# A fused mLSTM and gated feed-forward kernel on Trainium2: gate rows reordered for fewer transfers, and the first units rearranged

## The chip, the cores and the metric

The kernel runs on one core of one Trainium2 chip. The metric is the device time of the program in microseconds (us). Engines are named as in the profile: PE is TensorE (matmuls), DVE is VectorE, ACT is ScalarE, POOL is GpSimd, SP is SyncE, which here only issues DMAs. PE's clock has two levels in the profile: a granted clock of 1.00 is 2.4 GHz, 0.50 is 1.2 GHz.

## The reference

A gated linear attention (mLSTM) over 2 batches, 8 heads, 768 positions, head size 40, followed by two gated feed-forward layers with 320 model columns and 1536 hidden columns:

```
m_new = max(f + m, i);  f_stab = exp(f + m - m_new);  i_stab = exp(i - m_new)
C = f_stab * C + i_stab * v k^T;   n = f_stab * n + i_stab * k
y = sigmoid(o) * (C q) / max(|n.q|, 1)
x = y in token order, 1536 x 320
x = (silu(xn @ w_gate) * (xn @ w_val)) @ w_out      with xn = x / rms(x) * rms_g
x = (sigmoid(x @ w_gate2) * (x @ w_val2)) @ w_out2
```

All of it is in float32.

## The kernel before

**Tiles.** Time is cut into 6 chunks of 128 positions; with 2 batches this makes 12 attention tiles t of 128 tokens x 8 heads. Within a chunk the recurrence is written as matmuls: the exponents of the decay matrix come from one matmul of `lhs` (rows a) and `rhs` (rows log, spread over 4 heads), ACT takes the exponential into `prob`, PE makes the scores q k^T, DVE multiplies (`weigh_scores`), and PE multiplies with v (`outputs`). A state per batch is carried from chunk to chunk. `normalise(t)` divides and applies the output gate, `sum_squares` (ACT), `root` (POOL, a power of -0.5) and `scale_y` or `early_scale` make the normed x, `turn_x` (PE) transposes it, and `round_x` (ACT) and `rest_x` (DVE) split it in a high part `x_hi` and a rest `x_lo`.

**Gate rows.** The gates' prefix sums and maxima run along the free dimension, with one (batch, head) pair a partition: 16 rows, and a second copy of them for chunk 0. Each value goes into the exponent matmul as high part and rest. The gates are handled in three parts (`PARTS`): chunk 0, chunk 1, and chunks 2 to 5, which are copied to other partitions (`m_q`, `fi_q`, "late rows") so that one instruction handles four chunks. Their results come back by DMA: `load_lhs` writes a's rows into `lhs`, `load_rows(j)` the log rows of half tile j into one of four `rhs` buffers.

**Units.** The feed-forward work is cut into 78 units u, each 128 hidden columns by 256 or 512 tokens. In a unit PE runs `gate_products(u)`, `value_products(u)` and `result_products(u - 1)`; ACT applies the activation (`activate`) and rounds the hidden values (`round_hidden`); DVE does `gate_hidden` (units of the first two blocks), `value_hidden`, `rest_hidden`. PE starts gate_products(u + 1) only when `gate_hidden(u)` has read the bank. Units 0 to 11 have 256 tokens. Tiles 0 and 1 are made ahead of unit 0; tiles 2 to 11 are woven into the units: `SCORE_AT` starts tile 2 at unit 0, tile 3 at unit 2, tile 4 at unit 9, tile 5 at 11 and so on; `OUT_AT` is one unit later.

**Order.** No scheduler: each engine's order is that of the code, and semaphores join the engines. Each engine takes its instructions strictly in order, so one that waits holds up all behind it. `G2` is a table of the units at which the five steps for the late rows stand: stabiliser(2) on DVE; late_differences on POOL and the mask rows on ACT; late_sums and round_late; late_exponentials and late_rests; late_decays. SP's loads of them follow a unit later (`G2[0] + 1`, `G2[3] + 1`). `WARM` holds how many matmuls on a constant tile (`keep_clock_up`) stand at ten places ahead of unit 0.

**PE ahead of unit 0**: filling matmuls; scores(0); scores(1); early_exponents(0) to (3); early_outputs(0) to (3); turn_x(0); turn_x(1); turn_gates(0); filling matmuls between them.

Of the kernel before, what the change touches and what calls it, by code (L numbers as in the profile page):

```python
# [12 lines left out]
F32 = mybir.dt.float32  # L13
F32R = mybir.dt.float32r
# [52 lines left out]
LATE = B * H * (CH - C2)  # L67
EARLY = 8
G2 = (2, 4, 5, 5, 6)
WARM = (12, 0, 2, 0, 0, 5, 2, 4, 2, 1)  # L70
# [7 lines left out]
def pattern(j):  # L78

    return HG * (2 * (j // 2 % B) + j % 2)  # L80
# [22 lines left out]
def build(nc, qk1, k1, v1, og, fi_in, fi_late, gains, const, masks, wgv1, wo1, wgv2, wo2, outT):  # L103
    with ExitStack() as ctx:
# [27 lines left out]
        ones = sb("ones", [LATE, ROWS])  # L132
# [3 lines left out]
        is_a, is_log = consts[0:GATES, C_A:C_A + 1], consts[0:GATES, C_LOG:C_LOG + 1]  # L136
# [3 lines left out]
        with rows:  # L140
# [5 lines left out]
            c_gate = sb("c_gate", [B * H, CH], F32, rows)  # L146
            c_diag = sb("c_diag", [B * H, CH, B, H], F32, rows)
            log_early = sb("log_early", [ROWS, L], F32, rows)
            r_row = sb("r_row", [GATES, C2, L], F32, rows)
# [3 lines left out]
            c_q, diag_q = sb("c_q", [LATE, 1], F32, rows), sb("diag_q", [LATE, LATE], F32, rows)  # L153
            a_split = sb("a_split", [2 * LATE, L], F32, rows)
# [5 lines left out]
        with att:  # L160
# [9 lines left out]
            log_rows = sba("log_rows", [ROWS, 1, L])  # L170
            log_split = sba("log_split", [2 * LATE, L])
# [6 lines left out]
            gate = [sba(f"gate{p}", [P, H, D]) for p in range(2)]  # L178
            den, rden = sba("den", [P, H]), sba("rden", [P, H])
            y1 = sba("y1", [P, H, D])  # L180
            ssq, msq, rstd = (sba(n, [P, 2]) for n in ("ssq", "msq", "rstd"))
# [3 lines left out]
            mask_l = y_tail[ROWS:P, 0:2 * L].rearrange("p (m s) -> p m s", m=2)  # L185
# [12 lines left out]
        xt_ps = lambda t: (bank[4], bank[1])[t] if t < B else bank[7]  # L198
        cols_ps = lambda p: bank[7][:, H * DV + (2 * B * H if p == 1 else 0):]
# [5 lines left out]
        fi_late_in, m_late_in, ones_in, lhs_in = (sem(n) for n in ("fi_late_in", "m_late_in", "ones_in", "lhs_in"))  # L205
# [9 lines left out]
        m_done, kl_own, kl_done, log_done, a_own, a_done, log_hi_done, log_lo_done, a_hi_done, a_lo_done, w_done = (  # L215
            sem(n) for n in ("m_done", "kl_own", "kl_done", "log_done", "a_own", "a_done", "log_hi_done",
                             "log_lo_done", "a_hi_done", "a_lo_done", "w_done"))
        lhs_const, rhs_const, sel_const, setup_pool, im_done, exps_done, cols_turned, cols_done, diag_done, rhs_own, act_own = (
            sem(n) for n in ("lhs_const", "rhs_const", "sel_const", "setup_pool", "im_done", "exps_done", "cols_turned",
                             "cols_done", "diag_done", "rhs_own", "act_own"))  # L220
# [6 lines left out]
        gate_done, den_done, rden_done, y1_done, y_done, ssq_done, msq_done, rstd_done, xn_done = (  # L227
            sem(n) for n in ("gate_done", "den_done", "rden_done", "y1_done", "y_done", "ssq_done",
                             "msq_done", "rstd_done", "xn_done"))
# [18 lines left out]
        def _(sp):  # L248
# [7 lines left out]
            def load_rows(j):  # L256
# [7 lines left out]
                for n in range(2):  # L264
                    src = log_rows[GATES * n + at:GATES * n + at + HG, 0]
                    if c >= C2:
                        at_late = LATE * n + B * H * (c - C2) + at
                        src = log_split[at_late:at_late + HG]
                    sp.dma_start(rhs[i][GATES * n + B * H:GATES * n + B * H + 1].bitcast(F32),
                                 src).then_inc(rows_in[i], 16)  # L270

            def load_m_late():

                sp.wait_ge(m_done, 3)
                m = m_row[0:B * H].rearrange("p c s -> p (c s)")
                for c in range(C2, CH):
                    at = B * H * (c - C2)
                    sp.dma_start(m_q[at:at + B * H], m[:, L * c - 1:L * c + L]).then_inc(m_late_in, 16)
# [1175 lines left out]
```

## Time and profile before

| | |
|---|---|
| three timed runs | 494.49, 494.61, 496.36 us; median 494.61 us |
| profiled execution, its own time | 497.38 us |
| its span on the core | 495.6 us |
| mean granted clock | 0.985 |
| busy | PE 478.5 us (97%), DVE 228.3, ACT 185.8, POOL 29.9 |
| DMA | 26.08 MB, mean 53 GB/s |

PE is the engine to look at. Its busy time is modelled from the starts of pipelined matmuls, so its share says little alone; the stretches where it is idle, or where the granted clock is 0.50, are what can be won. A row of a timeline gives start, duration, engine, line, operation, output and inputs, and in square brackets the engine's idle time before it with what ended it.

### The profile page before, as it was taken

To read this page: it belongs to the slowest core of one execution; us is meant where nothing else is said; L and a number is where in the kernel's file an instruction comes from. 1 tells how busy PE (TensorE), PEld (TensorE's weight loads), DVE (VectorE), ACT (ScalarE), POOL (GpSimd) and SP (SyncE) were. 2 spreads that over 40 slices of the span, in tenths; PEclk is the share of its full clock that TensorE was granted. 3 is DMA by queue.
4 is the path that set the end of the run, shared out by engine and by line. 5 is a ranking of instruction groups with operands and counts; after the bars stand their busy time and mean duration, and the time that the engine had idled before them with its cause. 6 is when DMAs were issued, how large, how long until landed. Compare 5 with 4: busy or idle time off the path is not lost.

```text
span 495.6 us, 7191 instructions
## 1 busy us (share of the span) xinstructions
PE 478.5 (97%) x2700; PEld 397.9 (80%) x2702; DVE 228.3 (46%) x452; ACT 185.8 (37%) x386; POOL 29.9 (6%) x69
## 2 busy tenths in 40 slices
PE   8799889999999999999999999999999999999996
PEld 4599879888878877878888888888888888888884
DVE  4768736667555544454555545222232222322222
ACT  6645523554354242334545455122232212222221
POOL 3421101111101000000000000000000000000000
PEclk8979989999999999999999999999999999999999
DMA  6354215542020130000232320000010000100001
GB/s 206 124 154 136 82 22 170 159 128 67 1 69 18 37 118 0 2 1 1 63 117 91 92 76 0 2 0 1 0 54 1 0 1 0 54 1 0 1 1 53
DMA packets 15795, 26.08 MB, mean 53 GB/s; under 512 B 2448, under 2 KB 10736, under 8 KB 15760
## 3 DMA queue, kind: packets, MB, share of 16 engines
q1 hardware_dynamic: 15536, 25.50, 17.0%
q8 instruction: 21, 0.34, 0.3%
q10 hardware_dynamic: 224, 0.12, 0.1%
q14 instruction: 14, 0.11, 0.1%
HBM read 23.40 MB, written 1.97 MB: 51 GB/s over the span
## 4 chain that ended last, share of the span: by engine, by line
PE 57%; issue 34%; POOL 3%; DVE 2%; DMA 1%; ACT 1%; SPq 1%; POOLq 0%; ACTq 0%
PE bank L1257 37%; PE bank L1308 5%; PE bank L1310 5%; PE bank L1309 5%; PE bank L1316 2%; PE bank L1317 2%; POOL vw L438 1%; DMA qk_tile<-qk 1%; POOL msq L452 1%; POOL faded L445 1%; POOL rstd L455 1%; PE bank L1150 0%; PE bank L1191 0%; PE pair L1191 0%; DVE hid_lo L984 0%
## 5 line engine op out<-in xcount | busy, mean ns | idle before, releaser
L1257 PE MATMUL bank<-x_hi,gv_split 128*128 128x512 f32 (+1 forms) x780 | 242.1, 378 | 2.9 <-DVE x_lo L939 1.8
L1257 PE MATMUL bank<-x_lo,gv_split 128*128 128x512 f32 (+1 forms) x468 | 175.1, 377 | 0.0
L1257 PEld LDWEIGHTS bank<-x_hi,gv_split 128*128 128x128 f32 x780 | 145.6, 192 | 30.0 <-issue 3.8
L1257 PEld LDWEIGHTS bank<-x_lo,gv_split 128*128 128x128 f32 x468 | 89.7, 192 | 14.9
L582 ACT ACTIVATE hid_hi<-hid 128x512 fp32r<-128x512 f32 (+1 forms) x78 | 46.7, 599 | 140.4 <-DVE hid L977 90.5
L977 DVE TENSOR_TENSOR hid<-hid,bank 128x512 f32<-128x512 f32 x48 | 33.0, 688 | 132.4 <-PE bank L1257 132.4
L575 ACT ACTIVATE hid<-bank 128x512 f32<-128x512 f32 (+1 forms) x78 | 43.9, 562 | 112.5 <-PE bank L1257 112.4
L984 DVE TENSOR_TENSOR hid_lo<-hid,hid_hi 128x512 fp32r<-128x512 f32 (+1 forms) x78 | 51.3, 658 | 52.1 <-ACT hid_hi L582 52.1
L1308 PE MATMUL bank<-hid_hi,wo_split 128*128 128x512 f32 (+1 forms) x156 | 60.8, 389 | 0.4 <-DVE hid_lo L984 0.4
L1310 PE MATMUL bank<-hid_hi,wo_split 128*128 128x512 f32 (+1 forms) x156 | 58.3, 374 | 0.0
L1309 PE MATMUL bank<-hid_lo,wo_split 128*128 128x512 f32 (+1 forms) x156 | 58.3, 374 | 0.0
L1308 PEld LDWEIGHTS bank<-hid_hi,wo_split 128*128 128x128 f32 x156 | 29.4, 188 | 6.8 <-DVE hid_lo L984 0.8
L964 DVE SCALAR_TENSOR_TENSOR hid<-hid,bank 128x512 f32<-128x512 f32 (+1 forms) x30 | 17.4, 579 | 37.0 <-ACT hid L575 37.0
L1310 PEld LDWEIGHTS bank<-hid_hi,wo_split 128*128 128x128 f32 x156 | 29.4, 188 | 5.3
L1309 PEld LDWEIGHTS bank<-hid_lo,wo_split 128*128 128x128 f32 x156 | 29.4, 188 | 4.6
L1316 PE MATMUL bank<-hid_hi,wo_split 128*128 128x512 f32 (+1 forms) x78 | 29.2, 374 | 0.0
L1317 PE MATMUL bank<-hid_lo,wo_split 128*128 128x512 f32 (+1 forms) x78 | 29.1, 373 | 0.0
L973 DVE SCALAR_TENSOR_TENSOR hid<-hid,bank 128x512 f32<-128x512 f32 (+1 forms) x30 | 17.4, 580 | 22.3 <-PE bank L1257 21.6
L948 DVE TENSOR_TENSOR gv_split<-gv_raw,gv_split 128x768 fp32r<-128x768 f32 x24 | 23.2, 967 | 3.0 <-ACT gv_split L561 3.0
L1201 PEld LDWEIGHTS pair<-v_sb,prob 128*128 128x128 f32 x160 | 18.9, 192 | 0.4
L1201 PE MATMUL pair<-v_sb,prob 128*128 128x42 f32 x160 | 18.9, 279 | 0.0
L532 ACT ACTIVATE hsum<-gate 128x320 f32<-128x320 f32 x12 | 5.7, 474 | 29.8 <-DVE gate L923 29.8
(147 smaller groups left out, 376.3 us busy)
## 6 DMA issues: line engine op xcount, KB each, us to landing
gv_raw<-wgv SPq DMA_DIRECT2D x24, 384.0 KB, 3.1
qk_tile<-qk SPq DMA_DIRECT2D x24, 160.0 KB
wo_raw<-wo SPq DMA_DIRECT2D x24, 160.0 KB, 3.1
v_sb<-v SPq DMA_DIRECT2D x12, 168.0 KB, 4.3
gate<-og SPq DMA_DIRECT2D x12, 160.0 KB, 3.1
k_sb<-k SPq DMA_DIRECT2D x10, 160.0 KB, 4.3
outT<-y_out SPq DMA_DIRECT2D x6, 256.0 KB, 2.0
rhs<-log_split SPq DMA_DIRECT2D x32, 2.0 KB
```

The costliest lines, as they stand in the source:

```text
L575: ins = nc.scalar.activation(hid[j][:, 0:size], g_ps[:, 0:size], func, scale=0.5 if tanh else 1.0)
L582: nc.scalar.activation(hid_hi[j][:, 0:size], hid[j][:, 0:size], ACT.Copy).then_inc(hi_done, 1)
L948: nc.vector.tensor_tensor(wgv[f][:, :, 3:6], raw[:], wgv[f][:, :, 0:3].bitcast(F32), ALU.subtract).then_inc(gv_ready, 1)
L977: ins = nc.vector.tensor_tensor(h, h, v_ps[:, 0:size], ALU.mult)
L984: nc.vector.tensor_tensor(hid_lo[j][:, 0:size], hid[j][:, 0:size], hid_hi[j][:, 0:size].bitcast(F32), ALU.subtract).then_inc(lo_done, 1)
L1201: pe.matmul(pv_ps(2 * t + g)[:, DV * h:DV * h + DV], prob[t % 2][:, g, h], v_sb[t % 3][:, HG * g + h], start=True, stop=True)
L1257: mm = pe.matmul(ps[:, 0:size], lhs, rhs, start=(i == 0), stop=(i == len(passes) - 1))
L1308: pe.matmul(out, w_hi, hi, start=first, stop=False)
L1309: pe.matmul(out, w_hi, lo, start=False, stop=False)
L1310: mm = pe.matmul(out, w_lo, hi, start=False, stop=last)
L1316: pe.matmul(out, w_end, hi, start=first, stop=False)
L1317: mm = pe.matmul(out, w_end, lo, start=False, stop=last)
```

## The change

It reorders the gate rows, moves steps between engines, and moves steps along each engine's order. The arithmetic of the reference stays, with another split of the rounding.

1. **Gate rows.** The rows are now 32 (`GATES`) in four groups of (batch, half of the heads), and each group has its 4 heads twice: once for the a or log row's high part, once for its rest. So the two parts of a half tile stand next to each other, and `load_rows(j)` issues one DMA instead of two, `load_lhs` four instead of eight. The first gate load is one DMA instead of two. All gate instructions of part 1 handle 32 partitions instead of 16, those of the late rows 128 instead of 64.
2. **Late rows.** `G2` moves each step one unit later. SP loads the first chunk of `lhs`, then four rows, then the other chunks.
3. **Ahead of unit 0.** The exponents of tile 0 come before the scores of tile 1; early_outputs(0) comes before early_exponents(2). For tiles 0 and 1 the denominators' absolute value is taken on ACT (`magnitude`) instead of a second DVE instruction; tile 0's gate is raised by one on ACT and multiplied on POOL. `less_log` goes from POOL to DVE.
4. **x's tail.** The scaled x (384 columns, the last 64 of them twice) is written by one instruction that reads two overlapping windows of 192 columns, instead of two instructions; weights and gains are ordered to match. The mean's factor and the epsilon go into the square-sum (one more column, a scale), so `root` has one POOL instruction instead of two. Tile 1's transposes go to three banks, each with its own count.
5. **Units.** DVE does combine before rest_hidden; normalise comes behind the weights' rests in units 0 to 5. ACT does sum_squares one unit later, behind the exponential, where the next unit has scores.
6. `WARM` changes at six of its ten places; the filling matmuls ahead of unit 0 are 28 before and 29 after.

```diff
-LATE = B * H * (CH - C2)
+LATE = GATES * (CH - C2)
+GROUPS = B * 2
-G2 = (2, 4, 5, 5, 6)
-WARM = (12, 0, 2, 0, 0, 5, 2, 4, 2, 1)
+G2 = (3, 5, 6, 6, 7)
+WARM = (12, 0, 2, 1, 0, 8, 4, 4, 0, 0)
...
-            for n in range(2):
-                sp.dma_start(fi_row[B * H * n:B * H * n + B * H, :, 0], fi_in[:, :, 0]).then_inc(gates_in, 16)
+            sp.dma_start(fi_row[:, :, 0], fi_first).then_inc(gates_in, 16)
...
                 if u == G2[3] + 1:
-                    load_lhs()
+                    load_lhs(C2)
                     for j in range(4 * B, 4 * B + 4):
                         load_rows(j)
+                    for c in range(C2 + 1, CH):
+                        load_lhs(c)
...
+            def magnitude(t):
+                act.wait_ge(att_out, 2 * t + 2)
+                out = pv_ps(2 * t)[:, 0:H * DV].rearrange("p (h d) -> p h d", h=H)
+                nc.scalar.activation(den_abs[t][:], out[:, :, D], ACT.Abs, scale=2.0).then_inc(abs_done, 1)
...
+            def first_gating():
+                pool.wait_ge(y1_done, 1)
+                pool.wait_ge(gate_raised, 1)
+                nc.gpsimd.tensor_tensor(gate[0][:], gate[0][:], y1_first[:], ALU.mult).then_inc(y_first_done, 1)
...
             def root(t):
                 pool.wait_ge(ssq_done, t + 1)
-                need(pool, rstd_done, t - 1)
-                nc.gpsimd.tensor_scalar(mine(msq, t), mine(ssq, t), 1.0 / DM, 1e-6, ALU.mult, ALU.add).then_inc(msq_done, 1)
-                pool.wait_ge(msq_done, t + 1)
                 need(pool, xn_done, t - 1)
                 nc.gpsimd.tensor_tensor(mine(rstd, t), mine(msq, t), half_pow[:], ALU.pow).then_inc(rstd_done, 1)
...
+                if u - 1 in OUT_AT and squares_later(u - 1):
+                    sum_squares(OUT_AT[u - 1])
                 activate(u)
...
-            weight_rows(0)
             early_weigh(0)
             early_weigh(1)
+            dve.wait_ge(gates_rest_in, 16)
+            stabiliser(1)
             early_weigh(2)
             early_weigh(3)
-            dve.wait_ge(gates_rest_in, 16)
-            stabiliser(1)
+            weight_rows(0)
             normalise(0)
             normalise(1)
+            sum_logs(1)
+            less_log(1)
             early_scale(0)
-            sum_logs(1)
+            rest_logs(1)
+            early_scale(1)
             rest_gv(0)
-            early_scale(1)
-            rest_logs(1)
-            weight_rows(1)
             rest_x(0)
             rest_x(1)
+            weight_rows(1)
...
                 value_hidden(u)
-                rest_hidden(u)
                 if u in OUT_AT:
                     combine(OUT_AT[u])
+                rest_hidden(u)
...
                 for n in out:
                     rest_wo(n)
+                if u in OUT_AT and u < SPLIT:
+                    normalise(OUT_AT[u])
                 if u == G2[0]:
                     stabiliser(2)
...
             scores(0)
             keep_clock_up(WARM[1], True)
-            scores(1)
             early_exponents(0)
             early_exponents(1)
+            scores(1)
+            early_outputs(0)
             keep_clock_up(WARM[8], True)
             early_exponents(2)
             keep_clock_up(WARM[9], True)
             early_exponents(3)
-            keep_clock_up(WARM[2], True)
-            early_outputs(0)
+            early_outputs(1)
             keep_clock_up(WARM[3])
-            early_outputs(1)
             early_outputs(2)
```

On PE ahead of unit 0, behind the first filling matmuls; qk_tile are scores, rhs with lhs the exponents, v_sb with prob the outputs. Before:

```order
L1181 MATMUL pair<-qk_tile 128x128
L1150 MATMUL bank<-rhs,lhs 128x4x64 x4
L1134 MATMUL bank<-fill 128x512 x2
L1150 MATMUL bank<-rhs,lhs 128x4x64 x2
L1134 MATMUL bank<-fill 128x512
L1150 MATMUL bank<-rhs,lhs 128x4x64 x2
L1134 MATMUL bank<-fill 128x512 x2
L1191 MATMUL pair<-v_sb,prob 128x42 x8
L1191 MATMUL bank<-v_sb,prob 128x42 x8
L1134 MATMUL bank<-fill 128x512 x5
```

And in the changed kernel, from the last row of scores(0):

```order
L1219 MATMUL bank<-qk_tile 128x128 x8
L1188 MATMUL bank<-rhs,lhs 128x4x64 x4
...
L1219 MATMUL pair<-qk_tile 128x128
L1229 MATMUL pair<-v_sb,prob 128x42 x4
L1188 MATMUL bank<-rhs,lhs 128x4x64 x4
L1229 MATMUL pair<-v_sb,prob 128x42 x4
L1175 MATMUL bank<-fill 128x512
L1229 MATMUL bank<-v_sb,prob 128x42 x8
L1175 MATMUL bank<-fill 128x512 x8
```

The first four exponent matmuls stand ahead of tile 1's scores, and the first outputs ahead of the last four exponent matmuls.

On DVE in unit 3, the second unit with an attention output (tile 3): from combine (inter, hsum) to the next unit's first step. Before:

```order
L984 TENSOR_TENSOR hid_lo<-hid,hid_hi 128x256
L895 TENSOR_TENSOR inter<-pair,r_col 128x336
L899 TENSOR_TENSOR hsum<-pair,inter 128x336
L934 TENSOR_TENSOR state<-bank,faded 128x168
L910 TENSOR_SCALAR den<-hsum 128x8
```

In the changed kernel, from the same hid_lo, which now has inter and hsum ahead of it:

```order
L1021 TENSOR_TENSOR hid_lo<-hid,hid_hi 128x256
L971 TENSOR_TENSOR state<-bank,faded 128x168
L985 TENSOR_TENSOR gv_split<-gv_raw,gv_split 128x2x384
L991 TENSOR_TENSOR wo_split<-wo_raw,wo_split 128x64
L993 TENSOR_TENSOR wo_split<-wo_raw,wo_split 128x256
L944 TENSOR_SCALAR den<-hsum 128x8
L946 SCALAR_TENSOR_TENSOR den<-hsum,den 128x8
L950 RECIPROCAL rden<-den 128x8
L954 TENSOR_TENSOR y<-hsum,rden 128x320
L960 SCALAR_TENSOR_TENSOR gate<-gate,y 128x320
L758 SCALAR_TENSOR_TENSOR m_row<-fi_row,m_row 32x512
L1001 SCALAR_TENSOR_TENSOR hid<-hid,bank 128x256
```

combine stands ahead of hid_lo, the weights' rests ahead of normalise, and the long scan over chunks 2 to 5 (m_row), which stood at the end of unit 2, ahead of unit 4's gate_hidden (the last row).

On SP's queue, the loads around the late rows. Before:

```order
L278 DMA m_q<-m_row 16x129 x4
L254 DMA qk_tile<-qk 40x1024 x2
L294 DMA v_sb<-v 128x336
L303 DMA k_sb<-k 128x320
L298 DMA gate<-og 128x320 x2
L287 DMA lhs<-a_split 16x2x128 x8
L269 DMA rhs<-log_split 1x4x128 x8
L307 DMA gv_raw<-wgv 128x768 x2
```

In the changed kernel:

```order
L293 DMA m_q<-m_row 32x129 x4
L310 DMA gate<-og 128x320
L300 DMA lhs<-a_split 32x2x128
L285 DMA rhs<-log_split 2x4x128 x4
L300 DMA lhs<-a_split 32x2x128 x3
L319 DMA gv_raw<-wgv 128x768 x2
```

Sixteen DMAs stood between the late rows' results and the next weights, eight of them ahead of the first rhs row; now there are eight, one of them ahead of it.

## Rows read from the trace of the kernel before

**Rows 1.** Windows, PE alone: start:end, length, busy (count), granted clock, DMA share, GB/s.
```profile
6.40:9.60 3.20, 2.24 (x33) 1.00 1.03 254
9.60:13.00 3.40, 3.40 (x13) 0.50 0.99 365
18.00:23.20 5.20, 2.24 (x13) 1.00 0.02 4
23.20:30.05 6.85, 6.28 (x32) 0.51 0.21 66
68.70:74.40 5.70, 3.84 (x18) 0.71 0.13 24
100.00:225.00 125.00, 123.81 (x787) 1.00 0.15 44
```

**Rows 2.** Waits of PE, first 100 us: total, times, longest.
```profile
PE bank L1245 <- DVE swap L1014: 1.6, 1, 1.6
PE bank L1257 <- DVE x_lo L939: 1.6, 2, 1.0
...
PE pair L1181 <- ACT prob L521: 1.3, 2, 0.6
...
PE pair L1170 <- DMA lhs<-a_split: 1.1, 1, 1.1
PE bank L1257 <- DVE hid L964: 1.1, 2, 0.6
...
PE pair L1170 <- DMA rhs<-log_split: 0.7, 1, 0.7
```

**Rows 3.** Timeline up to unit 0's first gate product.
```profile
0.71 1.49 SPq L321 DMA_DIRECT2D fi_row<-fi_in  x2
...
4.10 0.41 DVE L732 TENSOR_TENSOR_SCAN m_row<-fi_row 32x128 f32<-32x128 f32 x1 [4.10 <-DMA fi_row<-fi_in]
...
9.61 1.22 PE L1150 MATMUL bank<-rhs,lhs 128*128 128x256 f32 x4
...
13.05 0.60 ACT L515 ACTIVATE prob<-bank 128x512 f32<-128x512 f32 x1 [0.28 <-PE bank L1150]
...
17.62 0.19 POOL L452 TENSOR_SCALAR msq<-ssq 128x1 f32<-128x1 f32 x1 [1.34 <-ACT hsum L532]
...
19.41 1.01 POOL L452 TENSOR_SCALAR msq<-ssq 128x1 f32<-128x1 f32 x1 [0.96 <-ACT hsum L532]
...
21.09 0.56 DVE L1013 TENSOR_SCALAR swap<-gate,rstd 128x320 f32<-128x320 f32 x1 [0.73 <-POOL rstd L455]
...
24.38 0.55 PE L1257 MATMUL bank<-x_hi,gv_split 128*128 128x256 f32 x1 [0.57 <-DVE x_lo L939]
```

**Rows 4.** Timeline, units 1 to 5.
```profile
31.64 0.39 PE L1257 MATMUL bank<-x_hi,gv_split 128*128 128x256 f32 x1
...
33.38 1.98 PE L1201 MATMUL pair<-v_sb,prob 128*128 128x42 f32 x16
...
38.87 0.16 DVE L910 TENSOR_SCALAR den<-hsum 128x8 f32<-128x8 f32 x1
...
40.03 0.49 DVE L923 SCALAR_TENSOR_TENSOR gate<-gate,y 128x320 f32<-128x320 f32 x1
...
46.58 1.27 DVE L732 TENSOR_TENSOR_SCAN m_row<-fi_row,m_row 16x512 f32<-16x512 f32 x1
...
54.76 0.36 PE L1257 MATMUL bank<-x_hi,gv_split 128*128 128x256 f32 x1 [0.60 <-DVE hid L964]
```

**Rows 5.** Timeline, SP's DMA issues for the late rows.
```profile
61.69 5.13 SPq L287 DMA_DIRECT2D lhs<-a_split  x8
...
67.34 5.21 SPq L269 DMA_DIRECT2D rhs<-log_split  x8
```

**Rows 6.** Timeline, PE, unit 13.
```profile
98.67 0.71 PE L1170 MATMUL pair<-rhs,lhs 128*128 128x256 f32 x4 [0.42 <-issue]
```

**Rows 7.** Waits of all engines, 80 to 230 us.
```profile
ACT hsum L532 <- DVE gate L923: 23.9, 8, 3.5
```

More of the change, by code:

```diff
@@ L460, in _ @@
             pool.wait_ge(consts_in, 16)
-            for i in range(4):
+            for i in range(2):
+                select_rows(i)
+            keep_logs(1)
+            for i in range(2, 4):
                 select_rows(i)
             less_m(1)
-            keep_logs(1)
+            first_gating()
             root(0)
             root(1)
-            less_log(1)
             pool.wait_ge(cols_done, 1)
@@ L526, in gate_tanh, with raise_gate @@
                 nc.scalar.activation(gate[t % 2][:], gate[t % 2][:], ACT.Tanh, scale=0.5).then_inc(gate_done, 1)
+            def raise_gate():
+                act.wait_ge(gate_done, 1)
+                act.wait_ge(setup_pool, 6)
+                nc.scalar.activation(gate[0][:], gate[0][:], ACT.Identity, bias=ones[:, 0:1]).then_inc(gate_raised, 1)
             def sum_squares(t):
-                act.wait_ge(y_done, t + 1)
-                need(act, msq_done, t - 1)
+                if t == 0:
+                    act.wait_ge(y_first_done, 1)
+                else:
+                    act.wait_ge(y_done, t)
+                act.wait_ge(setup_pool, 10)
+                need(act, rstd_done, t - 1)
@@ L626, in round_a @@
                     return
-                for m in range(2):
-                    nc.scalar.activation(lhs[0:GATES, c0:c1, m], a_row[:, c0:c1], ACT.Identity,
-                                         scale=is_a, bias=is_log).then_inc(a_hi_done, 1)
+                nc.scalar.activation(a_hi[:].bitcast(F32R), a_row[:, c0], ACT.Copy).then_inc(a_hi_done, 1)
             def gate_exponentials(p):
@@ L711, in _ @@
                     round_x(TURN_AT[u])
-                if u in OUT_AT:
+                if u in OUT_AT and not squares_later(u):
                     sum_squares(OUT_AT[u])
@@ L1384, in constants @@
     c[R:P, C_TAIL] = 1.0
[L1385 to L1391 removed]
+    second = np.arange(P) // HG % 2
+    c[:, C_A], c[:, C_LOG] = 1 - second, second
+    for n in range(GROUPS * HG):
+        first = n // HG * H + n % HG
+        for row in (first, first + HG):
+            c[row, C_SEL + n], c[GATES + row, C_SEL + n] = 1.0, -1.0
+        c[first, C_SEL_A + n], c[first + HG, C_SEL_A + n] = -1.0, 1.0
     return c
```

349 lines of the change are left out of this document (175 added, 174 removed).

## The prediction

> **What bounds the kernel now.** I read the windows first, then PE's waits, then the timeline at each of them. From 100 us on there is nothing to win: of 125.00 us PE is busy for 123.81 at full clock [rows 1], and the rest of the kernel is as dense. So what this change can do is in the first 100 us, where PE loses time in two ways: it waits, and the granted clock falls to 0.50 behind stretches in which it did little. There are three such falls. PE is busy for 2.24 of the 3.20 us up to 9.60 and runs at 0.50 for the next 3.40. It is busy for 2.24 of 5.20 us up to 23.20 and runs at about 0.51 for the next 6.85, the whole of unit 0. And in 68.70 to 74.40, where it waits for the late rows, the mean is 0.71 [rows 1]. The waits behind them are in the list [rows 2]: 1.6 us for tile 1's scaled x (`swap`), 1.6 for `x_lo`, 1.3 for the exponential `prob`, 1.1 for `gate_hidden`, and 1.1 + 0.7 for the DMAs of the late rows.
>
> My sum is made against the profiled execution, 497.38 us with a span of 495.6. The median of the timed runs is 494.61, or 2.77 lower; I take the gain over unchanged to the median.
>
> **Term 1: up to unit 0's first gate product, at 24.38 [rows 3].**
> - First gate load. Two DMAs take 1.49 us to issue, 0.75 each, and DVE's scan starts at 4.10 when the second has landed. One DMA: 0.75 earlier.
> - Exponents. They start at 9.61, behind tile 1's scores, which waited for their DMA. Ahead of the scores they need only their rows, which DVE and ACT have ready about 8.0, now 7.3, so they run at about 7.5. ACT is then the limit: it still spreads the fourth `rhs` and is free at about 8.7. Its four exponentials of 0.60 us cannot all follow at once, since the third argument matmul is queued behind early_outputs(0), and this behind DVE's first product, about 10.0. The last exponential comes at about 11.85 in place of 13.05: 1.2 earlier, with the 0.75 in it.
> - Normalising. From there, one DVE instruction goes to ACT, tile 0's gating to POOL, and `root` is one POOL instruction. The removed `msq` took 0.19 us for tile 0, but 1.01 for tile 1, where it stood beside DVE's split of a weight (an instruction with two inputs in SBUF). Tile 1's scaled x started at 21.09. Counted along the new order, ACT squares tile 1 by 17.2, POOL's power ends by about 18.2, `swap` is written by 18.8. In place of the end of `swap`'s second half at 21.8 this is 3.0 earlier: 1.2 from above, 0.8 from `msq`, 1.0 from the rest.
> - Behind it DVE now splits the first weight (about 0.9 us) ahead of rest_x(0), so x_lo is ready about as much later than `swap` as before. Unit 0's first gate product: 21.4 in place of 24.38, **3.0 us**.
>
> One doubt in this: POOL and DVE side by side. The two `msq` rows differ by 0.82 us for the same work [rows 3]. I have put 0.4 us into the sum for tile 0's power, which now meets DVE's gating, scan and less_log. The Trainium skill (SBUF — State Buffer, section "SBUF: two separate sides") has this as an exclusive lock: a DVE instruction with two SBUF inputs and a GpSimd one exclude each other for a whole instruction. The trace agrees by the 1.01 us. By that rule the 0.4 would be up to 1.0, if POOL waited out all three.
>
> **Term 2: unit 0 at full clock.** From its first gate product to unit 1's takes 31.64 - 24.38 = 7.26 us, nearly all at 1.2 GHz [rows 1, 4]. The stretch ahead of it now holds 8 + 4 + 4 filling matmuls in place of 5 + 2 + 4, and is about 3 us shorter. I expect no fall there. PE's own part would then halve to 3.5, but ACT's chain (columns' exponentials, weight split, activation, 1.0 us of exponential) ends first at about 24.8, so unit 1 starts at about 26.2 and its outputs, which start at 33.38 [rows 4], at about 27.7. **33.38 - 27.7 is 5.7 for terms 1 and 2 together, 2.7 of it the clock.** Had the clock the same fall, this 2.7 is gone.
>
> **Term 3: units 2 to 6, DVE's and ACT's order.** Two stalls on `prob` of about 0.6 each (1.3 in two [rows 2]): in unit 2 the exponential came behind sum_squares, and no longer does. But sum_squares now holds up activate(2), since normalise(2) has moved behind the weights' rests: it is ready some 1.6 us later (normalise takes from 38.87 to 40.52 [rows 4]). I count 0.8 us later for tile 3's outputs. In unit 3 DVE then has the 1.27 us scan [rows 4] ahead of gate_hidden(4), with combine's stretch 0.8 later: the gate product of unit 5, which today starts at 54.76 after a wait of 0.60, comes 2.1 later in the old time. The next wait, 1.0 on x_lo [rows 2], is hidden by that, and one of 0.5 on gate_hidden in unit 7 shrinks. At tile 4's exponents I count **1.25 us lost**. What the steps move ahead of is only work whose results are wanted later; its cover is PE's two units in flight, and it is gone when a step comes more than about a unit late, 3 us.
>
> **Term 4: the late rows.** Today SP issues eight lhs DMAs in 5.13 us and eight rhs DMAs in 5.21 [rows 5], 0.65 each; PE waits 1.13 and 0.73 us and the clock falls behind that. The results now come one unit later, about 65.5 in the old time, but PE needs only one lhs and two rhs DMAs: issued by 67.5, landed by 69.3, with the 1.8 us from issue to landing that the last rhs takes now (issue of the fourth at 69.3, PE at 71.06). PE arrives at 68.75 + 1.25 = 70.0. No wait. Saved are 1.9 of waiting, and the clock: 3.3 us of work at half speed behind it, 1.7. **3.6 us.** The margin is 0.7.
>
> **Term 5: later units.** The other 0.64 on `prob`, in unit 11, and 0.42 where tile 6's exponents waited for combine [rows 6], which now stands ahead of rest_hidden: **1.1 us**. The `x` windows save 0.2 on ACT per tile beside PE's work: nothing. Twice the partitions in an instruction costs nothing, as length is by elements of a partition; two loads grow by 64 KB and 80 KB in a stretch where DMA moves 254 to 365 GB/s [rows 1], 0.5 us at worst in what comes behind them, and that is ahead of its use by more.
>
> **Sum:** -5.7 + 1.25 - 3.6 - 1.1 = -9.15. Profiled 488.2, median 494.6 - 9.1 = **485.5 us**.
>
> **The rivals.**
> - A. *The clock falls all the same ahead of unit 0.* For it: there are still idle stretches of about 1.2 and 0.6 us between the fills, and PE waits for x_lo. Against: today's stretch has 3 of 5.2 idle. Term 2's 2.7 is lost: 488.2. Chance 0.2.
> - B. *The late rows are late again.* They start a unit later and the margin is 0.7; if late_sums waits for its inputs (scan at the end of unit 3, four DMAs, POOL), all comes later. Then about 1 us of wait and a fall worth 1.7: 488.2. Chance 0.13.
> - C. *Term 3 is not paid*: stalls of DVE and ACT there find more slack than I counted. 484.2 and down to 483 with more from term 1. Chance 0.15.
> - D. *Slower.* sum_squares now stands ahead of the next unit's activation, on an in-order engine. Today ACT waits 23.9 us in 8 tiles for the gated y, 3 us each, at a place where nothing else was due [rows 7]. If normalise ended later than the unit's own activation is due, each of ten tiles would pay. The loss has to reach 9.1 + 2.5 = 11.6 us, 1.16 a tile, for the kernel to be slower by more than 0.5%. Against it: from unit 6 normalise stands where it stood, and PE has two units' products in flight to cover it. With the price 1.5 a tile: 500.5. Chance 0.03.
> - E. *It does little*: terms 1 and 2 come to under 2 us since the first transfers set the pace (a DMA share of 1.03 and 0.99 up to 13 us [rows 1]), and A and B hold: about 493.5. Chance 0.05.
>
> The forecast itself has 0.44, from 484 to 487.5. The range takes A, B and most of C in, with both together at the edge: **482.8 to 491.0**. A measurement of this kernel tells about 0.5%, 2.5 us, from no change. Faster by more 0.90, within 0.05, slower 0.05.
>
> **What would show it.** Unit 0's first gate product at about 21.4 in the timeline, and a granted clock of 1.00 from 13 to 31 us; the last early exponential near 11.9. Unit 1's outputs near 27.7. A wait of gate products in unit 5 grown to 1.5 or more, and none on x_lo behind it. No wait on lhs or rhs DMAs near 62 us, and no fall there. No wait on `prob`. I am wrong if the clock falls behind the rearranged start (A), or if the list of waits has a new one on `hid` or DMA that is over 2 us.

## The result and the profile after

The changed kernel takes 486.76 us (median of four, 485.60 to 487.33) against 494.55 (four, 493.68 to 496.36): ratio 0.983, 95% interval 0.981 to 0.985. The forecast was 485.5 with a range of 482.8 to 491.0. The profiled execution took 485.60 us (span 483.8), 11.8 less than that of before. The ratios below leave out single executions over 1.5% above the fastest of their kernel, which is one of no_fills (496.50 us) and one of before (504.85).

The timeline of the changed kernel ahead of unit 0, against [rows 3]:

```profile
0.73 0.76 SPq L332 DMA_DIRECT2D fi_row<-fi_first  x1
3.29 0.41 DVE L758 TENSOR_TENSOR_SCAN m_row<-fi_row 32x128 f32<-32x128 f32 x1 [3.29 <-DMA fi_row<-fi_first]
...
7.95 0.74 PE L1188 MATMUL bank<-rhs,lhs 128*128 128x256 f32 x4
...
11.47 1.09 ACT L523 ACTIVATE prob<-bank 128x512 f32<-128x512 f32 x2 [1.80 <-PE bank L1188]
...
16.26 0.56 POOL L462 TENSOR_TENSOR rstd<-msq,half_pow 128x1 f32<-128x1 f32 x1 [0.67 <-ACT hsum L556]
...
17.58 0.71 POOL L462 TENSOR_TENSOR rstd<-msq,half_pow 128x1 f32<-128x1 f32 x1 [0.76 <-ACT hsum L556]
...
18.32 0.42 DVE L1052 TENSOR_SCALAR swap<-gate,rstd 128x384 f32<-128x384 f32 x1 [0.19 <-POOL rstd L462]
...
21.34 0.36 PE L1294 MATMUL bank<-x_hi,gv_split 128*128 128x256 f32 x1 [0.41 <-DVE x_lo L976]
```

The scan starts 0.81 earlier, the last of tile 0's and 1's exponentials starts at about 12.0, swap is written by 18.74, and the first gate product stands at 21.34. PE in the units behind it, at the places of [rows 4 to 6]:

```profile
28.11 1.98 PE L1239 MATMUL pair<-v_sb,prob 128*128 128x42 f32 x16
...
40.65 1.98 PE L1239 MATMUL pair<-v_sb,prob 128*128 128x42 f32 x16 [0.86 <-DVE prob L914]
...
50.90 0.36 PE L1294 MATMUL bank<-x_hi,gv_split 128*128 128x256 f32 x1 [1.61 <-DVE hid L1001]
...
63.58 0.64 PE L1208 MATMUL pair<-rhs,lhs 128*128 128x256 f32 x4
...
69.98 1.87 PE L1239 MATMUL pair<-v_sb,prob 128*128 128x42 f32 x16
...
88.66 0.64 PE L1208 MATMUL pair<-rhs,lhs 128*128 128x256 f32 x4
```

SP's issues for the late rows, against [rows 5]:

```profile
59.65 0.65 SPq L300 DMA_DIRECT2D lhs<-a_split  x1
60.40 2.83 SPq L285 DMA_DIRECT2D rhs<-log_split  x4
63.35 2.53 SPq L300 DMA_DIRECT2D lhs<-a_split  x3
```

Tile 4's exponents (63.58) have no wait in front. Two waits have grown, ahead of tile 3's outputs (0.86) and of unit 5's gate product (1.61). The clock, by windows of PE (start:end, length, busy (count), granted clock, DMA share, GB/s), against [rows 1]:

```profile
13.00:18.00 5.00, 3.63 (x24) 1.00 0.82 245
18.00:21.30 3.30, 2.92 (x16) 1.00 0.06 19
21.30:28.00 6.70, 6.57 (x82) 1.00 0.67 185
...
40.00:43.00 3.00, 2.35 (x20) 1.00 0.50 124
43.00:50.00 7.00, 6.29 (x70) 1.00 0.00 0
50.00:60.00 10.00, 9.02 (x74) 1.00 0.09 23
```

In this execution there is no fall left in these stretches. But the three timed ones had a mean clock of 0.991 where this one had 0.998, and took 1.2 to 1.7 us more. Before's profiled execution is the other way round: 0.985 and 2.8 us above its median.

### The profile page after: what moved, and what is told of

Read it like the earlier page. It is cut to its first block, busy times and chain, and to the rows that moved or that the text cites. A ratio compares the mean times of both kernels' runs of the same rounds, so it can differ in the third digit from the quotient of the medians.

```text
span 483.8 us, 7161 instructions
## 1 busy us (share of the span) xinstructions
PE 472.3 (98%) x2704; PEld 393.7 (81%) x2705; DVE 227.0 (47%) x447; ACT 184.4 (38%) x378; POOL 26.7 (6%) x59
## 4 chain that ended last, share of the span: by engine, by line
PE 87%; issue 5%; DVE 4%; ACT 3%; POOL 1%; DMA 1%; DVEq 0%; ACTq 0%; POOLq 0%
PE bank L1294 52%; PE bank L1345 7%; PE bank L1346 6%; PE bank L1347 6%; PE bank L1353 3%; PE bank L1354 3%; PE pair L1239 3%; PE pair L1219 2%; PE pair L1249 2%; PE pair L1208 1%; PE bank L1268 1%; DVE x_lo L976 1%; PE bank L1283 1%; DMA fi_row<-fi_first 1%; POOL rstd L462 0%
## 5 line engine op out<-in xcount | busy, mean ns | idle before, releaser
L1294 PE MATMUL bank<-x_hi,gv_split 128*128 128x512 f32 (+1 forms) x780 | 239.3, 375 | 2.8 <-DVE hid L1001 1.9
L1294 PE MATMUL bank<-x_lo,gv_split 128*128 128x512 f32 (+1 forms) x468 | 173.1, 373 | 0.0
L1294 PEld LDWEIGHTS bank<-x_hi,gv_split 128*128 128x128 f32 x780 | 143.3, 188 | 29.7 <-issue 3.4
L1294 PEld LDWEIGHTS bank<-x_lo,gv_split 128*128 128x128 f32 x468 | 88.0, 188 | 14.9
L1346 PEld LDWEIGHTS bank<-hid_lo,wo_split 128*128 128x128 f32 x156 | 29.4, 188 | 4.6
L1354 PEld LDWEIGHTS bank<-hid_lo,wo_split 128*128 128x128 f32 x78 | 14.7, 188 | 2.7
```

Of the source, the lines that this page charges most:

```text
L1294: mm = pe.matmul(ps[:, 0:size], lhs, rhs, start=(i == 0), stop=(i == len(passes) - 1))
L1346: pe.matmul(out, w_hi, lo, start=False, stop=False)
L1354: mm = pe.matmul(out, w_end, lo, start=False, stop=last)
```

## The experiments

Theory: the gain is the five terms of the prediction, and what is missing in the median comes from a clock fall behind one of the waits that term 3 makes. Rival: the fall is rival A's, ahead of or in unit 0, where the filling matmuls decide it. Times are medians; "at full clock" means executions with a mean clock of 0.998 to 1.000. Kernels stand in three groups that each share runs of before on one chip (median of before 495.96, 495.26, 495.0): the first has same_again and the three with other fills, the second normalise_first, squares_now, late_rows_early and lhs_all_first, the third scan_unit2, two_loads, pe_order_old and later_units_old. So the kernels of the third, which are built on normalise_first, were not run beside it.

### same_again: nothing edited

> The changed kernel once more, nothing edited. One profiled execution of it took 485.60 us at a mean clock of 0.998, three timed ones 486.75 to 487.33 at 0.991. Theory: the kernel has a clock fall that comes in some executions only, ahead of or in unit 0, and it costs 1.2 to 1.7 us. Then the times fall again in two groups, near 485.6 with a mean clock of 0.998 and near 487 with 0.991, and if the profiled execution is of the second group, a stretch at 0.50 of some 7 us stands ahead of 31 us. Rival: the time varies for another reason (a DMA that lands later), and the clock only follows; then a profile with 0.991 shows a wait of over 1 us that the first profile does not have, ahead of the fall.

Measured: 487.15 us (485.82 to 489.67), profiled 487.19 at 0.993, ratio 0.981 (0.976 to 0.986). Its waits and its windows:

```profile
40.70 1.98 PE L1239 MATMUL pair<-v_sb,prob 128*128 128x42 f32 x16 [0.87 <-DVE prob L914]
```

```profile
21.30:28.00 6.70, 6.53 (x82) 1.00 0.76 240
...
40.00:43.00 3.00, 2.30 (x19) 0.96 0.41 107
43.00:50.00 7.00, 7.00 (x53) 0.53 0.00 0
```

The two executions are alike within 0.05 us up to tile 3's outputs. Then one stays at 1.00 and the other is at 0.50 for 6.8 us. The fall is not ahead of unit 0 but behind the wait of 0.87 us, so the place in the expectation was wrong, and so was its rival: no extra wait stands ahead of it. It costs 1.6 us and not the 3.4 of its work, since the wait of 1.61 ahead of unit 5's gate product is gone behind it: PE reaches that product at 52.43, 1.53 later than it started in the first execution, and with no wait over 0.15.

### fills_old, no_fills, before_more_fills: filling matmuls alone

```diff
-WARM = (12, 0, 2, 1, 0, 8, 4, 4, 0, 0)
+WARM = (12, 0, 2, 1, 0, 5, 2, 4, 0, 0)    # fills_old
+WARM = (12, 0, 2, 1, 0, 0, 0, 0, 0, 0)    # no_fills
...
-WARM = (12, 0, 2, 0, 0, 5, 2, 4, 2, 1)    # kernel before
+WARM = (12, 0, 2, 0, 0, 10, 6, 6, 2, 1)   # before_more_fills
```

> The changed kernel with the filling matmuls of its last three places ahead of unit 0 at the counts of before, 5, 2, 4 in place of 8, 4, 4. Theory (term 2 of the prediction): the fills hold the clock; with five fewer the stretch from 13 to 21 us has more idle time, the clock falls before or in unit 0 in every execution, and the time is 1.5 to 2.7 us longer, 487.5 to 489.5. Rival: the stretch is short enough by itself, since it lost 3 us of idle time; then no change, 485.6 to 487.3, the first gate product at 21.3 to 21.5 and no stretch below 1.00 in unit 0.

> The changed kernel with no filling matmuls at the last three places ahead of unit 0 (0, 0, 0 in place of 8, 4, 4). The fills work on a constant tile and their results are not read. Theory: the clock falls behind 13 us and unit 0 runs at 0.50 for some 7 us, which costs 2.7 us as term 2 of the prediction has it; with the time of x's transposes at the low clock 488.5 to 490. Rival: the price of the fall is smaller, since ACT's and DVE's chains and not PE end last in unit 0: 487 to 488.

> The kernel before with more filling matmuls at the last three places ahead of unit 0, 10, 6, 6 in place of 5, 2, 4: the clock part of the change alone, without a shorter stretch. Theory (term 2): unit 0 runs at 1.00 and the kernel gains 2 to 2.7 us, 492 against 494.6. Rival: the fall comes from the waits between the fills (3 of 5.2 us idle, for swap and x_lo), which more fills at these places do not cover; then 494.6 and the clock at 0.51 behind 23.2 us as before.

fills_old: 486.6 us (485.59 to 487.59), as its rival had it. Two executions were at a clock of 1.00 with 485.6. The profiled one (0.989) took 487.54. It had the fall at 43 as well, and a shorter one ahead of and into unit 0 (0.71, and 0.72 up to 24.0), with tile 2's outputs at 28.58, 0.47 later than in the first profile of the changed kernel:

```profile
18.00:21.30 3.30, 3.30 (x15) 0.71 0.16 46
```

So the five added fills are worth nothing at full clock, and no difference of the medians can be told; whether they keep this short fall away in some executions is open.

no_fills: four executions between 488.23 and 496.50, ratio 0.990 (0.982 to 0.998); three of the four are above the 488.5 to 490 of the theory. The clock is low from within 13 to 18 us to the end of unit 0, and once more from 45.4 to 55.7:

```profile
13.00:18.00 5.00, 1.89 (x17) 0.67 0.83 256
18.00:21.30 3.30, 1.94 (x8) 0.50 0.04 14
21.30:28.00 6.70, 6.41 (x42) 0.50 0.76 242
...
43.00:50.00 7.00, 6.40 (x54) 0.67 0.15 45
50.00:60.00 10.00, 9.92 (x68) 0.72 0.09 23
```

The first gate product stands at 21.59, 0.20 later than in same_again, and tile 2's outputs at 31.05, 2.90 later. The 2.70 between the two are term 2's price of 2.7 for unit 0, which was right in size. Tile 3's outputs are still 2.90 later; behind them the fall lasts longer than that of same_again (10.2 in place of 6.8 us), and tile 4's exponents are 4.06 later.

before_more_fills: 494.18 (ten, 492.27 to 496.73), ratio 0.995 (0.992 to 0.998), 2.5 us by the ratio and 1.8 by the medians.

```profile
13.00:18.00 5.00, 5.00 (x34) 0.77 0.75 234
18.00:21.30 3.30, 3.30 (x13) 0.61 0.00 0
21.30:28.00 6.70, 6.36 (x38) 0.94 0.01 2
```

The clock from 21.3 to 28 us is 0.94, where [rows 1] had 0.51, but the first gate product comes at 26.30, 1.9 later than before, behind fills that run at a low clock. Tile 2's outputs start at 32.89, 0.49 earlier than the 33.38 of [rows 4]: that is what the fills bring where they stand, and not the 2 to 2.7 of the theory. The larger part of what this profile is ahead of before's comes elsewhere. Its waits for the late rows are those of before (1.12 and 0.73, for 1.13 and 0.73), but the clock behind them stays at 1.00, where before's was 0.71, and tile 4's outputs start 2.01 earlier than before's 78.70:

```profile
76.69 1.87 PE L1201 MATMUL pair<-v_sb,prob 128*128 128x42 f32 x16
```

Of these 2.01, 0.50 stood already ahead of the two waits. No fill stands near them. So a fall need not follow these waits, and where it does, it costs 1.5.

### normalise_first

```diff
-                if u in OUT_AT and u >= SPLIT:
+                if u in OUT_AT:
                     normalise(OUT_AT[u])
...
-                if u in OUT_AT and u < SPLIT:
-                    normalise(OUT_AT[u])
```

> The changed kernel with normalise ahead of the weights' rests in every unit, as in the kernel before, all else as changed. Two executions of the changed kernel are the same up to a wait of 0.86 us ahead of tile 3's outputs (40.65 us); behind it one stays at full clock and the other is at 0.50 for 7 us, and they end 1.6 us apart. Theory: this wait is term 3's (sum_squares(2) waits for normalise(2), and activate(2) stands behind it), and the fall in some executions hangs on it. Then with normalise(2) some 1.6 us earlier the wait is under 0.3, no execution has the fall, and the median is 1 to 2 us lower: 485 to 486, mean clock 0.998. Rival 1: the wait has another cause (the exponential itself, DVE's order), it stays at 0.8 and so do time and fall: 487. Rival 2: the weights' rests, now later, hold up PE in units 1 to 5: a new wait for gv_split or wo_split, 487 to 489.

484.58 us (six, 484.56 to 484.65), ratio 0.977 (0.974 to 0.981); all six at full clock, and a little below the 485 to 486 of the theory. Its timeline:

```profile
39.63 1.98 PE L1237 MATMUL pair<-v_sb,prob 128*128 128x42 f32 x16
...
48.15 1.27 DVE L758 TENSOR_TENSOR_SCAN m_row<-fi_row,m_row 32x512 f32<-32x512 f32 x1
49.34 0.38 DVE L1001 SCALAR_TENSOR_TENSOR hid<-hid,bank 128x256 f32<-128x256 f32 x1
...
49.87 0.36 PE L1292 MATMUL bank<-x_hi,gv_split 128*128 128x256 f32 x1 [1.60 <-DVE hid L1001]
```

The wait ahead of tile 3's outputs is gone, they start 1.02 earlier, and 1.02 is what remains at the end (484.58 against 485.60, both at full clock). So moving normalise behind the weights' rests, one part of the change, was a loss. All six executions are below the lowest of the changed kernel's eight (485.60), though those ran in other groups. The other wait stays at 1.60, and DVE's rows show why: the scan stands right ahead of gate_hidden.

### squares_now

```diff
             def squares_later(u):
-                return u + 1 in SCORE_AT and u + 1 not in ENDS
+                return False
```

> The changed kernel with sum_squares at the end of its own unit everywhere, as before. Theory (terms 3 and 5): ACT then stands at sum_squares(2), which waits for normalise(2) behind the weights' rests, with the exponential of tile 3 behind it; tile 3's outputs wait 1.5 us or more in place of 0.86, and in unit 11 the wait of 0.6 on prob is back: 1.3 to 2 us longer, 488 to 489. Rival (D of the prediction in a weak form): sum_squares ahead of the next unit's activation costs as much as it saves; then no change, 486 to 487.5.

491.7 us (nine, 487.43 to 492.37), ratio 0.990 (0.986 to 0.993); the two executions at full clock took 487.43 and 487.44. Its longest wait, and PE's windows behind it:

```profile
38.37 1.92 PE L1219 MATMUL pair<-qk_tile 40*128 40x128 f32 x16 [2.13 <-ACT prob L529]
```

```profile
38.00:40.00 2.00, 1.63 (x16) 0.64 0.87 258
40.00:42.00 2.00, 2.00 (x12) 0.50 0.50 164
```

At full clock the price is 1.8, as expected, and the wait stands ahead of tile 3's scores. The wait on `prob` in unit 11 is back too (0.76). The median pays 4.3 more, which the expectation did not have: five of the nine executions had a mean clock of 0.985 or 0.986. In the profiled one (0.993) the clock is low from 38.6 to 45.4.

### late_rows_early

```diff
-G2 = (3, 5, 6, 6, 7)
+G2 = (2, 4, 5, 5, 6)
```

> The changed kernel with the five steps for the late rows at the units of before (2, 4, 5, 5, 6 in place of 3, 5, 6, 6, 7). Theory: the long scan of 1.27 us then stands in unit 2 and not ahead of gate_hidden(4), so the wait of 1.61 us of unit 5's gate product falls to under 0.5; term 4 stays, since it comes from the fewer DMAs and their order, so no wait on lhs or rhs DMAs. About 1 us shorter, 485.5 to 486.5. Rival 1: the later units are what saves term 4 (the steps no longer meet the rest of units 4 and 5 on DVE and ACT); then other waits of 1 us come in units 3 to 6 and the time is 487 to 489. Rival 2: the wait in unit 5 is tile 3's lateness passed on, and stays with the scan moved: 487.

488.29 us (486.99 to 490.67), ratio 0.986 (0.981 to 0.991). The theory fell: the wait of unit 5 grew. DVE, ACT, then PE:

```profile
48.03 0.38 DVE L944 TENSOR_SCALAR den<-hsum 128x8 f32<-128x8 f32 x1
...
50.10 0.47 ACT L556 ACTIVATE hsum<-gate 128x321 f32<-128x321 f32 x1 [3.67 <-DVE gate L960]
...
50.56 0.36 ACT L598 ACTIVATE hid<-bank 128x256 f32<-128x256 f32 x1
...
51.53 0.36 PE L1294 MATMUL bank<-x_hi,gv_split 128*128 128x256 f32 x1 [2.08 <-DVE hid L1001]
```

The activation stands behind sum_squares, which waits 3.67 us for a late normalise: rival D's mechanism, in one unit. It is there in the changed kernel too (a wait of 3.44), where the activation is done at 50.12, only 0.25 before the scan lets gate_hidden start at 50.37. So the wait at 50.90 has two things stacked ahead of it, and without the scan it would shrink by some 0.2 (an estimate from these rows). That it grew by 0.47 has another cause, as this edit moves all five steps and not the scan alone: the late differences on POOL (47.08 to 48.75) now run beside DVE's work for normalise. Three DVE instructions there took 0.48, 0.38 and 0.33 us, against 0.22, 0.16 and 0.17 in the changed kernel.

### scan_unit2

On top of normalise_first:

```diff
-G2 = (3, 5, 6, 6, 7)
+G2 = (2, 5, 6, 6, 7)
```

> normalise_first (484.58 us, its six times within 0.1) with one step more: the long scan (stabiliser(2)) one unit earlier, at the end of unit 2, the other steps of the late rows where they are. In normalise_first the longest wait left in units 1 to 8 is 1.60 us on gate_hidden(4) at 49.87 us, and on DVE the scan's 1.27 us stand right ahead of it, while DVE waits 0.65 and 0.61 us for PE in unit 3. Theory: one unit earlier the scan is hidden by these two waits, the wait in unit 5 is 0.3 to 0.4, and the kernel is 1.2 us faster: 483.3 to 483.7. Rival 1: gate_hidden(3) comes 1.2 later behind the scan, and PE waits there in its place: 484.5. Rival 2: the wait is held by something else too (in late_rows_early, with the scan early, it was 2.08, behind sum_squares(3)); then it stays over 1 us: 484.3 to 484.6.

Profiled 483.69, lowest 483.40, both at full clock; median 485.28 (five), ratio 0.979 (0.977 to 0.981), since three executions had a mean clock of 0.987 to 0.993.

```profile
48.98 0.35 PE L1292 MATMUL bank<-x_hi,gv_split 128*128 128x256 f32 x1 [0.44 <-DVE hid L1001]
```

The wait fell by 1.16 us and the landmarks behind it are 0.89 earlier (ahead of it this execution was 0.28 later). So the size of the theory holds at full clock, and with it the two stacked causes: normalise_first takes the late normalise away and keeps 1.60 of wait, this kernel takes both. In the median it cannot be told from normalise_first, whose interval overlaps, and is not shown to beat it.

### lhs_all_first

```diff
-                    load_lhs(C2)
-                    for j in range(4 * B, 4 * B + 4):
-                        load_rows(j)
-                    for c in range(C2 + 1, CH):
+                    for c in range(C2, CH):
                         load_lhs(c)
+                    for j in range(4 * B, 4 * B + 4):
+                        load_rows(j)
```

> The changed kernel with SP's loads for the late rows in the order of before: all four chunks of lhs, then the four rhs rows. Theory (term 4): three DMAs of 0.65 to 0.84 us stand ahead of the rhs rows, PE waits 1.5 to 2 us for the rhs DMAs ahead of tile 4's exponents (63.6 us), and the clock may fall behind it: 488.5 to 490. Rival: halving the number of DMAs was all that mattered, the margin is wide enough and the order is worth nothing: 487, no wait on lhs or rhs.

488.77 us (487.06 to 491.8), ratio 0.986 (0.982 to 0.991).

```profile
65.42 0.47 PE L1207 MATMUL pair<-rhs,lhs 128*128 128x256 f32 x2 [0.61 <-DMA rhs<-log_split]
66.10 0.51 PE L1207 MATMUL pair<-rhs,lhs 128*128 128x256 f32 x2 [0.21 <-DMA rhs<-log_split]
```

The waits are back, 0.82 in an execution that had the fall at 43 and came late. By the times of the two executions at full clock (487.06 and 487.82 against 485.60) it is 1.5 and 2.2. No fall behind the waits in the profile. The order is worth 0.8 to 2.2 us; the 1.5 to 2 of waiting that I expected lies in that, but no profile at full clock shows it.

### two_loads, pe_order_old, later_units_old: on normalise_first

```diff
-            sp.dma_start(fi_row[:, :, 0], fi_first).then_inc(gates_in, 16)
+            for n in range(2):
+                half = slice(GATES // 2 * n, GATES // 2 * (n + 1))
+                sp.dma_start(fi_row[half, :, 0], fi_first[half]).then_inc(gates_in, 16)
...
-            dve.wait_ge(gates_in, 16)
+            dve.wait_ge(gates_in, 32)
```

> normalise_first with the first gate load as two DMAs of 16 rows, as in the kernel before (there 0.75 us each to issue). Theory (term 1): the scan starts 0.75 us later and all up to unit 0's first gate product with it (22.05 in place of 21.30), 485.2 to 485.5. Rival: part of it is taken back, since ACT's rows, PE's scores of tile 1 and the waits for DMAs behind it do not move: the first gate product under 0.4 later, 484.6 to 485.0.

```diff
+            scores(1)
             early_exponents(0)
             early_exponents(1)
-            scores(1)
-            early_outputs(0)
...
             early_exponents(3)
+            early_outputs(0)
             early_outputs(1)
```

> normalise_first with PE's order ahead of unit 0 as before: scores(1) ahead of the exponents, early_outputs(0) behind them. Theory (term 1, exponents): the first exponents wait behind scores(1) and its DMA, 1.0 us or more later than 7.95, and the last early exponential comes 0.4 to 1.2 us later; so does unit 0: 485.0 to 485.8, more if the clock falls behind the wait as it did before. Rival: ACT's four exponentials are the chain and the loads for scores(1) are there in time; then the first gate product stays at 21.3 to 21.5 and the time at 484.6 to 484.8.

```diff
                 value_hidden(u)
+                rest_hidden(u)
                 if u in OUT_AT:
                     combine(OUT_AT[u])
-                rest_hidden(u)
...
-                nc.scalar.activation(xn_of(t)[:, 0:3 * P].rearrange("p (w d) -> p w d", w=2), windows(t), ACT.Copy,
+                y = gate[t % 2][:].rearrange("p h d -> p (h d)")
+                nc.scalar.activation(xn_of(t)[:, 0:P + R], y[:, 0:P + R], ACT.Copy, scale=mine(rstd, t))
+                nc.scalar.activation(xn_of(t)[:, P + R:3 * P], y[:, P:DM], ACT.Copy,
+                                     scale=mine(rstd, t)).then_inc(xn_done, 1)
```

> normalise_first with two parts undone that can be told apart by their place: combine behind rest_hidden again, and scale_y as two instructions of 192 columns in place of one with two windows (the reading by windows of x's tail stays in tile 1's scale on DVE). Theory: combine is worth 0.4 us in unit 13 (term 5), a wait of 0.4 ahead of tile 6's exponents near 87.6; and the scale in one piece is worth up to 0.2 us in each of tiles 10 and 11, whose transposes had a wait of 0.46 on xn before and have none now: 485.0 to 485.4. Rival: the waits for xn went with the removed POOL instruction alone and combine has slack by now; then 484.6 and no new wait.

The profiled executions, all at full clock, against 484.58: two_loads 485.25 (+0.67; a second one at full clock took 485.69), pe_order_old 485.16 (+0.58), later_units_old 485.91 (+1.33, above the 485.0 to 485.4 of its theory). The medians are 487.13, 488.99 and 486.02. Executions at a mean clock of 0.985 to 0.993 are among them, in pe_order_old five of six. The first gate product of each of the first two, and in the third tile 6's exponents and tile 10's transposes:

```profile
21.95 0.36 PE L1294 MATMUL bank<-x_hi,gv_split 128*128 128x256 f32 x1 [0.40 <-DVE x_lo L978]
```

```profile
21.87 0.36 PE L1292 MATMUL bank<-x_hi,gv_split 128*128 128x256 f32 x1 [0.41 <-DVE x_lo L976]
```

```profile
88.04 0.71 PE L1208 MATMUL pair<-rhs,lhs 128*128 128x256 f32 x4 [0.41 <-issue]
...
186.63 0.55 PE L1283 MATMUL bank<-consts,xn 128*128 128x128 f32 x3 [0.18 <-ACT xn L565]
```

The first gate product of normalise_first stands at 21.30, so the single load and PE's order give 0.65 and 0.57 there, 1.2 together, and in these two executions all of it reaches the end. In the third, the wait of 0.41 in unit 13 is that of [rows 6], as term 5 had it. The waits on xn are back in tiles 10 and 11, and each moves what follows by 0.4. Both edits lie ahead of xn (combine in normalise's chain, the scale in ACT's), so their shares in this 0.8 are not told apart.

## Why the prediction was right, and where not

The total is inside the range by steps that mostly held; two errors of opposite sign hid in it: the sum was 2.6 us short of the gain between the two profiled executions, and carrying it over to the median took 4.0 us too much for granted. That the total lies 1.3 us from the forecast is partly luck. Measured between the two profiled executions, by what PE starts at the same place (tile 4's exponents before: 69.86 less their wait of 1.13, that is 68.73). Three places of before that were not shown:

```profile
45.62 1.88 PE L1201 MATMUL pair<-v_sb,prob 128*128 128x42 f32 x16
...
78.70 1.87 PE L1201 MATMUL pair<-v_sb,prob 128*128 128x42 f32 x16
...
197.82 0.55 PE L1245 MATMUL bank<-consts,xn 128*128 128x128 f32 x3 [0.46 <-ACT xn L540]
```

| term | up to | predicted | measured |
|---|---|---|---|
| 1 | unit 0's first gate product | 3.0 | 24.38 - 21.34 = 3.04 |
| 1 + 2 | tile 2's outputs | 5.7 | 33.38 - 28.11 = 5.27 |
| 3, part | tile 3's outputs | -0.8 | 45.62 - 40.65 = 4.97, so -0.30 |
| 3, part | unit 5's gate product | -2.1 | 54.76 - 50.90 = 3.86, so -1.41 |
| 3 | arrival at tile 4's exponents | -1.25 | 68.73 - 63.58 = 5.15, so -0.12 |
| 4 | tile 4's outputs | 3.6 | 78.70 - 69.98 = 8.72, so 3.57 |
| 5 | tile 6's exponents | 1.1 | 98.67 - 88.66 = 10.01, so 1.29 |
| not in the sum | the end | 0 | 11.78 - 10.01 = 1.77 |
| sum | | 9.15 | 11.78 |

- **Term 1** held in total and nearly in its parts: 1.2 for the load and the exponents (0.65 and 0.57 when undone), though the last early exponential came at about 12.0 and not at 11.85. The doubt about POOL beside DVE came out small: the two powers took 0.56 and 0.71 us. Of the ten later ones seven took 0.55, so the 0.4 put in for the first was hardly paid; the longest, 0.86 at 49.92, ran beside DVE's scan. The Trainium skill (SBUF — State Buffer, section "SBUF: two separate sides") would have allowed up to 1.0, with POOL waiting for whole instructions of DVE; these two rows show 0.16 at most.
- **Term 2** held in its mechanism: no fall ahead of or in unit 0 in either profile of the changed kernel. The 2.7 for it agrees with the 2.70 of no_fills; between the two profiles it was 5.27 - 3.04 = 2.23, as tile 2's outputs came at 28.11 and not at 27.7. That the shorter stretch carried it and not the added fills is argued from before_more_fills and fills_old, and the profile of the latter, with 0.71 ahead of unit 0, keeps it from being shown.
- **Term 3** named both stalls, their places and causes (the waits came out at 0.86 and 1.61). This is the term of the sum that was mis-sized: -1.25 predicted, -0.12 measured. Tile 3's outputs were only 0.30 late and not 0.8, for the old wait of 0.65 on `prob` went as the new one came. From there to unit 5 it was 1.11 for 1.3 (the wait grew from 0.60 to 1.61), and behind unit 5 1.29 came back, for 0.85. The 0.43 that terms 1 and 2 fell short hid part of this.
- **Term 4** held, 3.57 for 3.6: no wait and no fall. The order of the loads alone is worth 0.8 to 2.2 of it. But the 1.7 in it for the clock is a gain over this execution of before only: before_more_fills has the same waits, no fall behind them, and gets 1.5 of it without the change.
- **Term 5** held for units 11 and 13. That twice the partitions cost nothing held too: the scan takes 1.27 us for 16x512 [rows 4] and for 32x512. What the sum left out are the waits for xn in tiles 10 and 11, 0.46 each (the row above); after, neither is there. That is 0.9 of the 1.77. later_units_old brings 0.8 back with combine and the scale as before, so "the `x` windows save 0.2 on ACT per tile beside PE's work: nothing" may be where it failed, but the two edits were not undone apart. The rest of the 1.77 is not assigned.
- **From profile to median.** This is the step that failed most: "I take the gain over unchanged to the median". The profiled pair differs by 11.8 us, the medians by 7.8. Before's profiled execution had a mean clock of 0.985, where its executions beside the three groups of experiments had 0.969 to 0.996, with medians of 0.988, 0.992 and 0.992; the changed kernel's had the highest clock of its four. The fall behind its late rows, which before_more_fills lacks, may be part of that; how many executions of before had it was not seen. Rival A came true in another place: five of the changed kernel's eight executions had a mean clock of 0.991 to 0.993 and one had 0.983, and in the one of these that was profiled the clock falls at 43 us, behind term 3's wait, and costs 1.6.

Left open: what makes the clock fall in one execution and not in the next. normalise_first, without the wait ahead of tile 3's outputs, had a mean clock of 0.998 or more in all six executions. But the four kernels built on it lack that wait too, and 13 of their 21 executions had a mean clock of 0.985 to 0.993. Their profiled executions were all at full clock, so the place of those falls was not seen. Shown is the 1.02 us of the wait itself; that the fall hangs on it is not. The rearrangement of tile 1's transposes and `magnitude` were not undone either, so term 1's remaining 1.8 rests on the rows alone. Nor was the halved number of late DMAs tried apart from their order.

## What to carry to other kernels

Before a step is moved behind others on an in-order engine, look for the next engine that has a step waiting for it with the main work queued behind: normalise behind the weights' rests cost 1.02 us through sum_squares and the activation behind that. When two causes stand in front of one wait, taking one away may leave most of it: without the late normalise the wait stayed at 1.60, without both it was 0.44. And a step moved earlier can slow what it then runs beside, as the late differences on POOL did; read the rows on each engine in the chain. Last, compare profiled executions only with their mean clocks beside them: a gain read between two single executions was 4 us larger than that of the medians.

## What the runs showed of the hardware

- The granted clock is not a function of the program. Two executions with the same waits up to 43 us, within 0.05 us, went on at 1.00 and at 0.50 (for 6.8 us). The Trainium skill (TensorE: Matmul & The Clock Gate, section "Part 1: The HAM clock gate (the "warmup" mystery)") says that the monitor behind the clock runs free and does not start anew with a kernel, which would let one program meet it differently each time; no run here can show that.
- A fall costs only the work that has no wait behind it to give way: in same_again 3.4 us of lost work cost 1.6 of time, and the wait of 1.61 in unit 5 was gone. In the profile of squares_now the low stretch (38.6 to 45.4) lies ahead of tile 3's outputs, on which that wait hangs; the wait stays at 1.60, and the execution took 3.2 us more than those at full clock, for 3.4 of lost work.
- DVE pays beside POOL as well. In the changed kernel's tile 1, the 8-column step of normalise ran beside POOL's gating and took 0.37, against 0.17 for the same step of tile 0 with POOL idle. It ended at 15.62, right behind POOL's instruction (14.72 to 15.59). The 0.38 of late_rows_early is the same step: it ended at 48.41, POOL's at 48.38. The rows of the changed kernel:

```profile
13.71 0.17 DVE L942 TENSOR_SCALAR den<-den_abs 128x8 f32<-128x8 f32 x1
...
15.25 0.37 DVE L942 TENSOR_SCALAR den<-den_abs 128x8 f32<-128x8 f32 x1 [0.60 <-ACT den_abs L536]
```
